# Attention inside a split-precision matmul kernel: the products of weights and values, three steps back to back in place of two

## The chip, the cores and the metric

One core of a Trainium2 chip. The time is that of the device for one launch, in microseconds (us); a time of a kernel is the median of its runs. A profiled execution is one such run whose instructions were recorded. Engines are called PE (matrix), ACT (scalar), DVE (vector), POOL (GpSimd) and SP (which only issues DMAs here).

## The reference

Three layers follow each other. All is float32.

```python
# attention: q, k, v are (4 batches, 8 heads, 576 positions, 64)
scores = q @ k.T / 8 + bias          # bias: -slope * distance
mask = (rel >= 0) & (rel < 128)      # a query sees itself and the 127 keys before it
attn = softmax(where(mask, scores, -1e9))
x = attn @ v                         # -> (2304 tokens, 512)
# first block: 512 -> 1536 -> 512
x = (sigmoid(x @ w_gate) * (x @ w_val)) @ w_out
# second block: 512 -> 1024 -> 1024 -> 512
y = ((x @ w1) * (x @ w2)) @ w3 @ moe2_w_out
```

The kernel multiplies `w3` by `moe2_w_out` first (the fold), so that the second block ends in one product.

## The kernel before

**The dense work.** Tokens are taken in three thirds of 768. Every factor is split into a high and a low part in a reduced float format, and a product is three matmuls in that format (lines 610 to 612: high by high, low by high, high by low). Each weight matrix comes in groups of 256 columns, 6 groups for the first block and 4 for the second, so 30 groups in all. A group is multiplied by seven products in place of eight (P1 to P7, issued in the order P1, P5, P6, P2, P7, P3, P4; each is 6 matmuls), whose results DVE puts together in four pieces C11, C22, C12, C21. PE's work after the head is a list of 90 **sections**, numbered 0 to 89 here: `gate` and `val` for each group (the seven products with the gate weights, then with the value weights), and `proj` (or `pair0` and `pair1` at a block's end), in which the hidden result of the group before is multiplied by the output weights, in tiles of 6 matmuls. Within a block the sections run gate, val, gate, val, proj, gate, val, proj, and so on: sections 2, 5, 8, 11, 14 are gates, 3, 6, 9, 12, 15 vals, 4, 7, 10, 13 projs.

**The attention.** It is cut into 80 steps of 128 queries (some of 64) of two heads. A step n passes through a chain over all engines: `scores(n)` on PE (line 633), `score` on DVE, `exponentials` on ACT, `reciprocals` on DVE, `normalise` on POOL, `turn(n)` on PE, which turns the weights (line 648), `turned_copy(n)` into the place `pt[n % 2]` (DVE in the head, ACT later), `pv(n)` on PE (line 668), the product of turned weights and values, and `out_copies` on ACT (line 810) into the token matrix `xf`. The first 28 steps (`HEAD`) run in a head of 32 **slots** beside the fold, a step in each slot: scores(s), turn(s - 3). The other 52 run inside sections: step 28 + sec has its scores at the start of section sec, is turned in section sec + 1 (after P5, or after the second tile).

**Where pv stands.** Two steps are multiplied at a time. In the head pv(n - 1) and pv(n) stand at the start of slot n + 4 for odd n, and in the sections pv(m - 1) and pv(m) in section m + 1 - 28 for odd m, after P7 or after the sixth tile. So every even section holds a pair. The matmuls of pv are plain float32 and use 64 columns of the array for each of the two heads; all others use 128. A step of 64 queries also uses 64 rows of the array in half of its matmuls. The trace shows each float32 matmul of pv and scores as two instructions, so a full pair is 16.

**What it waits for.** In the sections `attn[0]` is the bank for scores and for the results of pv, so scores(n) waits for the copies of the pair before (`x_ready`), and ACT makes them in its own order: in a gate section between the pieces C11 and C22 of the gate, in a val section after the first `hidden_hi`. In a gate section ACT's chain is exponentials, turned_copy, `out_hi` (the output weights' high part, which waits for a DMA), a table load for the sigmoid, then gate(C11). P1 of the val section behind it waits for gate(C11), since they share a bank.

**DVE in a val section** makes the results and the hidden pieces in a fixed order, result_21 (line 1055) last, which is followed by hidden(C21), and its low part; the third tile of a proj or pair0 section waits for what stands at the end of that order.

**SP** issues all loads in program order. `load_v(j)` waits until the pv that read the old values is done, and whatever is behind it waits too.

## Time and profile before

| | |
|---|---|
| median of 3 runs | 885.34 us (883.81 to 888.36) |
| the profiled execution | 886.31 us |
| its span, first to last instruction | 884.5 us |
| PE busy | 864.6 us, 98% of the span |
| DVE, ACT, POOL busy | 515.2, 475.0, 594.9 us |
| matmuls of pv (line 668) | 576 instructions, in 40 groups |

The profiled execution took 0.97 us more than the median. The span lacks 1.8 us of it, which lie around the program. PE is granted full clock from about 22 us on. Its matmuls overlap, so a small wait doesn't show as idle time; what a piece of PE's work takes is read from the starts of the instructions around it.

### The profile page before, as it was taken

How to read it: one execution, taken by the hardware profiler on the slowest of the kernel's cores; microseconds unless marked ns; L12 is line 12 of the kernel's file. 1: busy time of each engine (PE TensorE's matmuls, PEld its weight loads, DVE VectorE, ACT ScalarE, POOL GpSimd, SP SyncE). 2: the span in 40 equal slices, each digit the busy share in tenths (PEclk: the TensorE clock that was granted, in tenths of full speed). 3: DMA queues.
4: the chain of work that ended last, by engine and by line, in shares of the span. 5: the costliest groups of instructions: out<-in, count | busy, mean ns of one | idle time of the engine just before them, and what ended most of it. 6: DMA issues, size and time to landing. Idle time of an engine off the chain costs nothing.

```text
span 884.5 us, 15389 instructions
## 1 busy us (share of the span) xinstructions
PE 864.6 (98%) x5272; PEld 825.7 (93%) x5272; DVE 515.2 (58%) x1209; ACT 475.0 (54%) x1043; POOL 594.9 (67%) x502
## 2 busy tenths in 40 slices
PE   5999999999999999999999999999999999999998
PEld 4887899999999999999999999999999999999998
DVE  5464656555467646656456656555676555576554
ACT  5566575666655644668555575633544444445330
POOL 3449588666655986758766663896859866738930
PEclk8999999999999999999999999999999999999999
DMA  8465323304222133331332122222221222212202
GB/s 243 123 197 161 113 93 103 92 15 117 91 79 82 35 104 98 100 126 52 96 109 88 48 81 80 72 72 72 80 102 46 84 72 72 72 49 72 72 24 73
DMA packets 59453, 78.79 MB, mean 89 GB/s; under 512 B 23152, under 2 KB 40688, under 8 KB 59376
## 3 DMA queue, kind: packets, MB, share of 16 engines
q1 hardware_dynamic: 58432, 77.52, 27.8%
q8 instruction: 43, 0.70, 0.3%
q10 hardware_dynamic: 944, 0.30, 0.1%
q14 instruction: 34, 0.28, 0.1%
HBM read 70.98 MB, written 6.82 MB: 88 GB/s over the span
## 4 chain that ended last, share of the span: by engine, by line
PE 80%; DVE 4%; ACT 4%; POOL 4%; issue 3%; DMA 2%; SPq 1%; ACTq 0%; DVEq 0%; POOLq 0%
PE quad_ps L610 14%; PE quad_ps L612 13%; PE quad_ps L611 13%; PE o_ps L610 11%; PE o_ps L612 10%; PE o_ps L611 10%; PE attn_ps L668 4%; PE attn_ps L633 3%; PE attn_ps L648 2%; DMA wo_lo_raw<-w_out 1%; DVE h_lo L1071 1%; PE quad_ps L633 1%; PE quad_ps L648 1%; POOL wq_lo L1280 1%; POOL wq_lo L1273 1%
## 5 line engine op out<-in xcount | busy, mean ns | idle before, releaser
L610 PE MATMUL quad_ps<-xs_hi,wq_hi 128*128 128x384 f32 x840 | 291.6, 347 | 3.2 <-DVE quad_ps L1043 1.8
L612 PE MATMUL quad_ps<-xs_hi,wq_lo 128*128 128x384 f32 x840 | 281.5, 335 | 0.0
L611 PE MATMUL quad_ps<-xs_lo,wq_hi 128*128 128x384 f32 x840 | 281.3, 335 | 0.0
L610 PE MATMUL o_ps<-h_hi,wo_hi 128*128 128x384 f32 x480 | 166.3, 347 | 3.0 <-DVE h_lo L1071 2.4
L610 PEld LDWEIGHTS quad_ps<-xs_hi,wq_hi 128*128 128x128 f32 x840 | 157.8, 188 | 10.3 <-issue 3.9
L612 PE MATMUL o_ps<-h_hi,wo_lo 128*128 128x384 f32 x480 | 161.3, 336 | 0.0
L611 PE MATMUL o_ps<-h_lo,wo_hi 128*128 128x384 f32 x480 | 161.1, 336 | 0.0
L611 PEld LDWEIGHTS quad_ps<-xs_lo,wq_hi 128*128 128x128 f32 x840 | 158.0, 188 | 0.0
L612 PEld LDWEIGHTS quad_ps<-xs_hi,wq_lo 128*128 128x128 f32 x840 | 157.7, 188 | 0.0
L1236 POOL TENSOR_TENSOR soft<-soft,recip 128x384 f32<-128x384 f32 (+2 forms) x80 | 58.3, 729 | 145.4 <-DVE recip L985 145.3
L1280 POOL TENSOR_TENSOR wq_lo<-wsum,wq_hi 128x1024 fp32r<-128x1024 f32 x60 | 144.3, 2405 | 8.5
L1273 POOL TENSOR_TENSOR wq_lo<-raw_q,wq_hi 128x768 fp32r<-128x768 f32 x60 | 110.7, 1845 | 52.4 <-ACT wq_hi L834 52.4
L1082 DVE TENSOR_TENSOR xf<-o_ps,xf 128x384 f32<-128x384 f32 x144 | 80.0, 556 | 65.9 <-PE o_ps L612 64.3
L1032 DVE TENSOR_TENSOR u<-quad_ps,s 128x384 f32<-128x384 f32 x60 | 33.4, 557 | 138.6 <-PE quad_ps L612 138.6
L868 ACT CAST h_hi<-quad_ps 128x384 fp32r<-128x384 f32 x120 | 57.6, 480 | 101.6 <-DVE quad_ps L1066 101.6
L610 PEld LDWEIGHTS o_ps<-h_hi,wo_hi 128*128 128x128 f32 x480 | 90.1, 188 | 8.5 <-issue 8.3
L611 PEld LDWEIGHTS o_ps<-h_lo,wo_hi 128*128 128x128 f32 x480 | 90.2, 188 | 0.0
L612 PEld LDWEIGHTS o_ps<-h_hi,wo_lo 128*128 128x128 f32 x480 | 90.1, 188 | 0.0
L848 ACT COPY s<-quad_ps 128x384 f32<-128x384 f32 x60 | 28.8, 481 | 110.5 <-PE quad_ps L612 110.5
L1286 POOL TENSOR_TENSOR wo_lo<-wo_lo_raw,wo_hi 128x1024 fp32r<-128x1024 f32 x30 | 71.6, 2394 | 19.2 <-ACT wo_hi L842 19.2
L797 ACT ACTIVATE soft<-soft,negmax 128x192 f32<-128x192 f32 (+1 forms) x144 | 62.0, 432 | 36.0 <-DVE negmax L975 35.8
L860 ACT ACTIVATE sig<-quad_ps 128x384 f32<-128x384 f32 x120 | 57.0, 495 | 35.0 <-DVE quad_ps L1049 14.7
(68 smaller groups left out, 1365.4 us busy)
## 6 DMA issues: line engine op xcount, KB each, us to landing
raw_q<-w SPq DMA_DIRECT2D x24, 512.0 KB, 3.7
raw_q<-w_gate SPq DMA_DIRECT2D x18, 512.0 KB, 3.6
raw_q<-w_val SPq DMA_DIRECT2D x18, 512.0 KB, 4.6
wo_lo_raw<-w_out SPq DMA_DIRECT2D x18, 512.0 KB, 4.2
wo_lo_raw<-w_times_wout SPq DMA_DIRECT2D x12, 512.0 KB, 3.8
w_raw<-w3t SPq DMA_DIRECT2D x16, 256.0 KB, 3.2
outT<-xf SPq DMA_DIRECT2D x8, 384.0 KB, 3.8
q_sb<-qT SPq DMA_DIRECT2D x30, 96.0 KB, 3.5
```

The costliest lines, as they stand in the source:

```text
L610: pe.matmul(out, lh, rh, start=start, stop=False, skip_group_check=onto)
L611: pe.matmul(out, lh, rl, start=False, stop=False, skip_group_check=onto)
L612: return pe.matmul(out, ll, rh, start=False, stop=stop, skip_group_check=onto)
L633: mm = pe.matmul(score_cols(n, u), q_sb[st][:, w], k_sb[st][:, keys], start=True, stop=True)
L797: op = nc.scalar.activation(soft_cols(n, u), soft_cols(n, u), ACT.Exp, scale=-1.0, bias=negmax[:, at + u:at + u + 1], accum_out=rowsum[:, ...
L860: nc.scalar.activation(sig[:, piece(blk)], quad[BANK_OUT[blk]][:, 0:TH], func).then_inc(gated, 1)
L868: nc.scalar.copy(h_hi[g % 2][:, piece(blk)], quad[BANK_OUT[blk]][:, 0:TH]).then_inc(h_hi_done, 1)
L1082: op = nc.vector.tensor_tensor(out=place, in0=ps_o[t % 2][:, 0:TH], in1=place, op=ALU.add)
L1236: nc.gpsimd.tensor_tensor(out=cols, in0=cols, in1=recip[:, at:at + units].unsqueeze(2).to_broadcast([P, units, UW - lo]), op=ALU.mult).the ...
L1273: nc.gpsimd.tensor_tensor(out=wq_lo[m][:, 0:PLAIN], in0=raw_q[m][:, GW:GW + PLAIN], in1=wq_hi[m][:, 0:PLAIN], op=ALU.subtract).then_inc(wq ...
L1280: nc.gpsimd.tensor_tensor(out=wq_lo[m][:, PLAIN:7 * GW], in0=wsum[m][:, :], in1=wq_hi[m][:, PLAIN:7 * GW], op=ALU.subtract).then_inc(wq_sp ...
L1286: nc.gpsimd.tensor_tensor(out=wo_lo[g % 2][:, :], in0=wo_raw[g % 2][:, :], in1=wo_hi[g % 2][:, :], op=ALU.subtract).then_inc(wo_split, 1)
```

## The change

pv is issued for three steps at a time. The new lists `VALUES` (the groups of three, counted anew from step 28, the last group of each stretch with one step) say which, and where: a group stands in the slot or section in which its last step's pv stood before. A third buffer `pt` holds turned weights. In the head a group has a bank of its own, alternating; in the sections its three results lie side by side in `attn[0]`. ACT's `out_copies` copies three, and SP's `load_v` stands where its group of three is done.

```diff
+VALUES = [list(range(a, min(a + 3, end))) for lo, end in ((0, HEAD), (HEAD, NSTEP)) for a in range(lo, end, 3)]
+VALUES_AT = {ns[-1]: i for i, ns in enumerate(VALUES)}
+VALUES_OF = {n: i for i, ns in enumerate(VALUES) for n in ns}
...
-        pt = [sb(ctx, f"pt{b}", [P, 4 * P], F32) for b in range(2)]
+        pt = [sb(ctx, f"pt{b}", [P, 4 * P], F32) for b in range(3)]
...
-            bank, start = (attn[n % 2], 0) if n < HEAD else (attn[0], n % 2 * 2 * UW)
+            bank = attn[VALUES_OF[n] % 2] if n < HEAD else attn[0]
+            start = (n - VALUES[VALUES_OF[n]][0]) * P
...
-                    if s == end_of(before(j, v_set)) + LAG_PV:
+                    if s == values_end(before(j, v_set)) + LAG_PV:
                         load_v(j)
...
-                    if end_of(before(j, v_set)) > HEAD and sec == end_of(before(j, v_set)) + 1 - HEAD:
+                    if end_of(before(j, v_set)) > HEAD and sec == values_end(before(j, v_set)) + 2 - HEAD:
                         load_v(j)
...
-                    pe.wait_ge(x_ready, n - 1 if n == HEAD else (n - 1) // 2 * 2)
+                    pe.wait_ge(x_ready, VALUES[VALUES_OF[n - 1]][0])
...
-                if 0 <= s - LAG_PV < HEAD and s % 2:
-                    pv(s - LAG_PV - 1)
-                    pv(s - LAG_PV)
+                if s - LAG_PV in VALUES_AT:
+                    for n in VALUES[VALUES_AT[s - LAG_PV]]:
+                        pv(n)
...
-                        if j == P7 and m is not None and m % 2:
-                            pv(m - 1)
-                            pv(m)
+                        if j == P7 and m in VALUES_AT:
+                            for n in VALUES[VALUES_AT[m]]:
+                                pv(n)
...
-                for n in (last - 1, last):
+                for n in VALUES[VALUES_AT[last]]:
                     nc.scalar.copy(out_cols(n), pv_cols(n)).then_inc(x_ready, 1)
...
-                wait(act, pv_done, n - 1)
-                nc.scalar.copy(cols(pt[n % 2]), cols(turn_bank(n))).then_inc(pt_done, 1)
+                wait(act, pv_done, n - 2)
+                nc.scalar.copy(cols(pt[n % 3]), cols(turn_bank(n))).then_inc(pt_done, 1)
```

The waits of pv itself follow: in the head for the copies two groups back, in the sections for those of the group before and for DVE's reading of the scores that share the bank.

On PE in the head, slots 5 and 6: before, the first two steps are multiplied (`attn_ps<-pt,v_sb`) in slot 5, after the scores (`quad_ps<-k_sb,q_sb`) and ahead of the transposes (`quad_ps<-eye,soft`).

```order
L633 MATMUL quad_ps<-k_sb,q_sb 128x192
L668 MATMUL attn_ps<-pt,v_sb 64x128 x6
L648 MATMUL quad_ps<-eye,soft 128x128 x4
L610 MATMUL o_ps<-wo_hi,w_hi 128x512
L611 MATMUL o_ps<-wo_lo,w_hi 128x512
```

Now slot 5 goes from scores to transposes:

```order
L645 MATMUL quad_ps<-k_sb,q_sb 128x192
L660 MATMUL quad_ps<-eye,soft 128x128 x4
L622 MATMUL o_ps<-wo_hi,w_hi 128x512
L623 MATMUL o_ps<-wo_lo,w_hi 128x512
L624 MATMUL o_ps<-wo_hi,w_lo 128x512
L645 MATMUL quad_ps<-k,q 128x64
L645 MATMUL quad_ps<-k,q 128x128
L681 MATMUL attn_ps<-pt,v_sb 64x128 x10
L660 MATMUL quad_ps<-eye,soft 128x128 x4
```

and three steps stand in slot 6. From there a group comes every third slot.

On ACT in sections 2 to 4 (gate, val, proj of the second group): `sig` is the gate's pieces, `h_hi` the hidden ones, `pt` the turned copy, `xf<-attn_ps` the copies of pv's results. Before:

```order
L860 ACT_TABLE_LOAD
L860 ACTIVATE sig<-quad_ps 128x384
L810 COPY xf<-attn_ps 128x128 x2
L860 ACTIVATE sig<-quad_ps 128x384 x3
L848 COPY s<-quad_ps 128x384
...
L836 CAST wq_hi<-wsum 128x1024
L868 CAST h_hi<-quad_ps 128x384 x3
...
L836 CAST wq_hi<-wsum 128x1024
L810 COPY xf<-attn_ps 128x128 x2
```

and now:

```order
L873 ACT_TABLE_LOAD
L873 ACTIVATE sig<-quad_ps 128x384 x4
L861 COPY s<-quad_ps 128x384
...
L849 CAST wq_hi<-wsum 128x1024
L881 CAST h_hi<-quad_ps 128x384
L823 COPY xf<-attn_ps 128x128 x3
L881 CAST h_hi<-quad_ps 128x384 x2
```

The copies left the gate section and the proj section and stand in the val section between them, as pv does on PE. This goes on: groups stand in sections 3, 6, 9, up to 51, and one of a single step in 52, where pairs stood in 2, 4, 6, up to 52. In the first block all of them are val sections.

## Rows read from the trace of the kernel before

**Rows 1.** PE in order: start us, length us, engine, line, operation, count; section 8.

```profile
177.83 0.34 PE L612 MATMUL quad_ps<-xs_hi,wq_lo 128*128 128x384 f32 x1
...
179.41 0.33 PE L611 MATMUL quad_ps<-xs_lo,wq_hi 128*128 128x384 f32 x1
```

**Rows 2.** PE in order, around a pair of 12 instructions, section 16.

```profile
253.06 0.34 PE L612 MATMUL o_ps<-h_hi,wo_lo 128*128 128x384 f32 x1
...
254.42 0.34 PE L611 MATMUL o_ps<-h_lo,wo_hi 128*128 128x384 f32 x1
```

**Rows 3.** PE in order: pairs with a step of 64 queries, sections 26 and 32.

```profile
345.19 1.03 PE L668 MATMUL attn_ps<-pt,v_sb 128*64 128x128 f32 x16
...
402.34 1.18 PE L668 MATMUL attn_ps<-pt,v_sb 128*64 128x64 f32 x16
```

**Rows 4.** PE in order, head: a slot without a pair, one with it.

```profile
44.78 0.49 PE L633 MATMUL quad_ps<-k,q 128*128 128x192 f32 x2
...
45.24 0.48 PE L610 MATMUL o_ps<-wo_hi,w_hi 128*128 128x512 f32 x1
...
61.75 0.49 PE L633 MATMUL quad_ps<-k,q 128*128 128x192 f32 x2
...
63.38 0.48 PE L610 MATMUL o_ps<-wo_hi,w_hi 128*128 128x512 f32 x1
```

**Rows 5.** PE in order, third tile of sections 4, 13 and 46; in brackets idle time and releaser.

```profile
136.78 0.41 PE L610 MATMUL o_ps<-h_hi,wo_hi 128*128 128x384 f32 x1
...
221.18 0.60 PE L648 MATMUL attn_ps<-eye,soft 128*128 128x128 f32 x4
221.53 0.42 PE L610 MATMUL o_ps<-h_hi,wo_hi 128*128 128x384 f32 x1
...
526.63 0.60 PE L648 MATMUL attn_ps<-eye,soft 128*128 128x128 f32 x4
527.61 0.41 PE L610 MATMUL o_ps<-h_hi,wo_hi 128*128 128x384 f32 x1 [0.39 <-DVE h_lo L1071]
```

**Rows 6.** DVE in order: result_21 at the end of sections 12 and 45.

```profile
219.13 0.55 DVE L1055 TENSOR_TENSOR quad_ps<-quad_ps,u 128x384 f32<-128x384 f32 x1
...
525.86 0.56 DVE L1055 TENSOR_TENSOR quad_ps<-quad_ps,u 128x384 f32<-128x384 f32 x1
```

**Rows 7.** PE in order: scores and the first product or tile behind, sections 7, 12.

```profile
162.20 0.81 PE L633 MATMUL attn_ps<-k_sb,q_sb 128*128 128x192 f32 x4
162.71 0.47 PE L610 MATMUL o_ps<-h_hi,wo_hi 128*128 128x384 f32 x1
...
208.48 0.81 PE L633 MATMUL attn_ps<-k_sb,q_sb 128*128 128x192 f32 x4
...
209.35 0.41 PE L610 MATMUL quad_ps<-xs_hi,wq_hi 128*128 128x384 f32 x1
```

**Rows 8.** SP and ACT in order: loads of section 10 and 11, ACT in section 11.

```profile
197.78 0.38 SPq L480 DMA_DIRECT2D v_sb<-v  x1
...
200.29 0.33 SPq L513 DMA_DIRECT2D wo_lo_raw<-w_out  x1
...
206.35 1.05 ACT L842 CAST wo_hi<-wo_lo_raw 128x1024 fp32r<-128x1024 f32 x1 [2.20 <-DMA wo_lo_raw<-w_out]
```

**Rows 9.** ACT and PE in order: the end of section 2.

```profile
124.33 0.49 ACT L860 ACTIVATE sig<-quad_ps 128x384 f32<-128x384 f32 x1
...
125.30 0.68 PE L633 MATMUL attn_ps<-k_sb,q_sb 128*128 128x64 f32 x4 [0.22 <-ACT xf L810]
125.73 0.42 PE L610 MATMUL quad_ps<-xs_hi,wq_hi 128*128 128x384 f32 x1
```

**Rows 10.** ACT and PE in order: sections 8 and 9.

```profile
178.01 0.49 ACT L860 ACTIVATE sig<-quad_ps 128x384 f32<-128x384 f32 x1
...
181.69 0.42 PE L610 MATMUL quad_ps<-xs_hi,wq_hi 128*128 128x384 f32 x1
```

**Rows 11.** PE in order, head, slot 28: a fold that waits.

```profile
81.13 0.50 PE L610 MATMUL o_ps<-wo_hi,w_hi 128*128 128x512 f32 x1 [0.59 <-POOL w_lo L1297]
```

More of the change, by code:

```diff
@@ L218, in starts_batch, with values_end @@
     return JOBS[j][3] == 0 and i == 0
+VALUES = [list(range(a, min(a + 3, end))) for lo, end in ((0, HEAD), (HEAD, NSTEP)) for a in range(lo, end, 3)]
+VALUES_AT = {ns[-1]: i for i, ns in enumerate(VALUES)}
+VALUES_OF = {n: i for i, ns in enumerate(VALUES) for n in ns}
+def values_end(j):
+    return VALUES[VALUES_OF[end_of(j) - 1]][-1]
 def chunks_of(n):
@@ L656, in pv @@
                 pe.wait_ge(pt_done, n + 1)
+                steps = VALUES[VALUES_OF[n]]
                 if n < HEAD:
-                    wait(pe, x_ready, n - 1)
+                    wait(pe, x_ready, VALUES[VALUES_OF[n] - 1][0] if VALUES_OF[n] else 0)
                 else:
-                    pe.wait_ge(x_ready, n // 2 * 2)
-                    pe.wait_ge(scored, min(n // 2 * 2 + 3, NSTEP))
+                    pe.wait_ge(x_ready, steps[0])
+                    pe.wait_ge(scored, min(steps[-1] + 2, NSTEP))
                 for c in chunks_of(n):
                     rows = slice(0, rows_of(n) if c == 1 else P)
-                    right = pt[n % 2][rows, c * 2 * P:(c + 1) * 2 * P].rearrange("p (u h n) -> p u h n", u=2, h=2)
+                    right = pt[n % 3][rows, c * 2 * P:(c + 1) * 2 * P].rearrange("p (u h n) -> p u h n", u=2, h=2)
                     for h in range(2):
@@ L785, in _ @@
                             turn(m)
-                        if i == 5 and m is not None and m % 2:
-                            pv(m - 1)
-                            pv(m)
+                        if i == 5 and m in VALUES_AT:
+                            for n in VALUES[VALUES_AT[m]]:
+                                pv(n)
         @block.scalar
@@ L882, in _ @@
             for s in range(SLOTS + 1):
-                if 0 <= s - LAG_PV - 1 < HEAD and s % 2 == 0:
+                if s - LAG_PV - 1 < HEAD and s - LAG_PV - 1 in VALUES_AT:
                     out_copies(s - LAG_PV - 1)
@@ L931, in _ @@
                     gate(g, C11)
-                    if m is not None and m % 2:
+                    if m in VALUES_AT:
                         out_copies(m)
@@ L939, in _ @@
                     hidden_hi(g, C11)
-                    if m is not None and m % 2:
+                    if m in VALUES_AT:
                         out_copies(m)
@@ L948, in _ @@
                         weights_hi(g + 1, 1)
-                    if m is not None and m % 2:
+                    if m in VALUES_AT:
                         out_copies(m)
@@ L955, in _ @@
                     x_hi(inst, P5)
-                    if m is not None and m % 2:
+                    if m in VALUES_AT:
                         out_copies(m)
@@ L960, in _ @@
                 else:
-                    if m is not None and m % 2:
+                    if m in VALUES_AT:
                         out_copies(m)
@@ L990, in turned_copy @@
                 dve.wait_ge(turned, n + 1)
-                wait(dve, pv_done, n - 1)
-                nc.vector.tensor_copy(cols(pt[n % 2]), cols(turn_bank(n))).then_inc(pt_done, 1)
+                wait(dve, pv_done, n - 2)
+                nc.vector.tensor_copy(cols(pt[n % 3]), cols(turn_bank(n))).then_inc(pt_done, 1)
             def fold_copy(m):
```

## The prediction, made before the changed kernel had run

> **What bounds the kernel now.** First the busy shares: PE is busy in 98% of the span, every other engine in 67% or less (the table above), so the time is PE's own work and the few places at which it waits. Then PE in order of time, and in it the distance from one start to the next, because matmuls overlap and the idle time in brackets shows only a part of a wait. The dense products start every 0.17 us without a break; the reader is to look for the larger distances. They are of two kinds. One kind stands at both ends of each group of pv, always of the same size. The other comes where PE waits for DVE, ACT or POOL, in different sizes, and depends on where a pair of pv gives the other engines time. The change touches both: there are 28 groups in place of 40, and most of them stand elsewhere.
>
> **A group's fixed price in the sections.** From the last product before a pair of 16 instructions to the second product behind it are 1.58 us [rows 1]; two ordinary distances of 0.17 would be 0.35, so the pair costs 1.23. A pair of 12 takes 1.36 [rows 2], so 1.01. The difference, 0.22 for four instructions, is 0.055 for each; 16 of them are 0.88, and 0.35 remain that don't depend on how many there are. Of these 0.10 lie ahead of the group and the rest inside its start, at its end, and at the product behind. Groups in sections fall from 26 to 18: 8 x 0.35 = 2.8 us less. All of it is PE's own time and nothing hides it. The Trainium skill speaks against this term: its page "TensorE: Matmul & The Clock Gate", section "Step-by-step: what each phase is for", says that the engine pulls weight loads ahead of the matmuls in flight, so that one matmul should follow another without a gap. By that page of the Trainium skill alone a group would have no price of its own, and without this term and its part in the head the sum would be 882.9. The Trainium skill's page "TensorEngine Tiling (Array Packing)", section "Key Properties", says on the other side that changing the tiling mode drains the engine, and pv is the only work in 64 columns.
>
> **In the head.** From scores to the first fold are 0.46 us without a pair (44.78 to 45.24) and 1.63 with one of 16 (61.75 to 63.38) [rows 4]; less 0.88 that leaves 0.29, say 0.3 for each group. They fall from 14 to 10.
>
> **Steps of 64 queries** cost more where another step follows in the group: 1.18 against 1.03 us [rows 3], 0.15. Of the 16 such steps 8 were last in their pair, and 6 are last in their group of three (or alone): two more pay, one in the head and one in the third third, 0.3 us.
>
> **Waits behind val sections.** In the third tile of a proj or pair0 section PE waits for the end of DVE's order. Where the val section held a pair, four transposes and the next product start 0.35 apart (221.18 to 221.53); in section 46, behind a val section without one, 0.98 (526.63 to 527.61), so the wait is 0.63. There are seven such, in sections 4, 10, 16, 28, 34, 40 and 46, from 0.32 in the first (136.78) to 0.63 in the last, together 2.6 us [rows 5]. The cause is a backlog of DVE: result_21 starts 2.05 us ahead of the transposes in the one (219.13) and 0.77 ahead in the other (525.86) [rows 6]. pv gives PE something to do after P7, while DVE catches up. Now each of the seven val sections in front holds a group of three, which gives more time than a pair. The backlog that would have to be left for a wait to return is 1.3 us; I take all 2.6 us as gone. What ACT adds in such a section is one more copy (two fit between the gate piece's end at 124.82 and the scores that wait for them at 125.30 [rows 9], so at most 0.24 us for one), behind the group and ahead of two hidden pieces, and P3 and P4 (12 x 0.17 = 2.1 us) hide it.
>
> **Waits at the start of val sections.** P1 waits for the gate piece C11 in sections 6, 12 and 36. In section 12 scores and product start 0.87 apart in place of 0.51 [rows 7]: 0.36. The other two, read in the same way, are 0.09 and 0.58; together 1.0 us. ACT was late because the output weights came late: it waited 2.20 us for them [rows 8]. SP had issued the new values at 197.78, when pv of its own section was done (in the others it waits for the section before), and the loads behind them, gate weights and output weights, went out together, so that the latter took 6.1 us from 200.29 to 206.35. Now every load of values waits for a group in the section before SP's place, in this place and in the two like it. I take the 1.0 us as gone.
>
> **What is lost: the cover in gate sections.** Nine gate sections held a pair and hold none now: 2, 8, 14, 20, 26, 32, 38, 44 and 50. There the pair's 1.23 us lay between ACT's gate C11 and the P1 that waits for it. In section 8 the piece ends at 178.50 and P1 starts at 181.69, 3.2 us later [rows 10]: without the pair 2.0 remain. In 14, 20, 26, 38, 44 and 50 the same reserve, from 1.7 to 4.1 us, also covers 1.23, in section 50 barely. Not in the sections after a block's start, 2 and 32, where ACT is behind: the piece ends at 124.82, P1 starts at 125.73 [rows 9], a reserve of 0.9. In section 2 PE also waits 0.39 now for the copies ahead of scores (125.30 [rows 9], read from the starts as above), and this wait goes. So PE would come 1.23 + 0.39 = 1.6 us earlier, and 0.7 of it is waited for again, 0.9 with 0.15 for the handing over: a loss of 0.5 against now. In section 32 the same sum gives 1.3 - 0.9 + 0.15 = 0.5. Together 1.0 us.
>
> **The head as a whole.** Up to slot 28 four groups are saved (12 to 8), 1.2 us, less 0.15 for a step of 64 queries. But there a fold waits for POOL [rows 11], which has worked almost without a break since slot 22 and won't be earlier because PE is; it starts its run on scores that come about 1.2 us earlier (three groups of 0.3, less 0.15, and one step's pv, 8 x 0.055, that now stands later). So the head gains 1.1 or 1.2 us, not more; 1.1 is taken. It could be nothing if POOL's run starts with a load or with ACT.
>
> **Two edits with one answer.** The third `pt` place and the other bank columns add no instruction. The loads of values are as many as before and come up to two steps later, with at least two groups between a load and the product that needs it; PE waits for none now.
>
> **The sum.** -2.8 (sections) + 0.15 (one step of 64 queries; the other is in the head's term) - 2.6 - 1.0 + 1.0 - 1.1 = -6.4 us. The profiled execution, 886.31, would be 879.9; it lies 0.97 above the median of 885.34, so the forecast is **878.9 us**, 0.7% less.
>
> **The rivals.** (a) Only the fixed price goes. The waits behind val sections move on to something else that is late at the same place (ACT, which has three copies, or POOL's low parts), and only 2.8 + 1.1 - 0.15, less the 1.0 lost, come: -2.8, 882.6 us. For it speaks that the waits are small against chains of several engines; against it that sections 7, 13, 25, 37 and 43, which already follow a val section with a pair, show none. (b) The gate sections lose their cover altogether. If the output weights still come late, as in section 11, the sigmoid ends just before P1 in each of the nine sections, and all of the pair's 1.23 us is waited for: 11 us in place of the 1.0 above, so 878.9 + 10 = 889 us, slower. It decides from the point at which the weights land 2 us later than they do in section 8. Against it speaks that the loads there are issued in the same order after the change as before. (c) More goes than I count: in section 52 the transposes wait 0.6 us for POOL, and a longer section 51 may cover it; in the head PE also waits for a copy of the pair before, and now waits for older ones. All of it together is -8.0, 877.3 us.
>
> **How the numbers follow.** The forecast with its neighbours (c) has 0.72, (a) 0.22, (b) 0.06. The range holds (a) and (c) with one us for the runs' own spread (the three of before lie between -1.5 and +3.0 of their median): 876 to 883.2. About 0.5%, 4.4 us, is what a measurement of this kernel can tell from no change. The forecast lies 6.4 below, (a) 2.8: faster 0.72, within 0.5% 0.23, slower 0.05.
>
> **What would show it.** 28 groups of pv, each with 0.35 us of its own: a group of 24 instructions should take 0.35 + 24 x 0.055 = 1.67 us between products. The third tiles of sections 4, 10, 16, 28, 34, 40 and 46 start 0.14 or 0.35 behind the transposes. P1 of sections 6, 12 and 36 starts 0.51 after scores; P1 of sections 3 and 33 waits 0.5 to 0.9, which no section did there before. The fold in slot 28 still waits for POOL. I am wrong if waits of that kind stand in the sections 9, 15, 21, 27, 39, 45 or 51 too (the cover was worth more than I read), or if the third tiles still wait for DVE (the backlog isn't what pv clears), or if a group of three costs more at its ends than a pair.

## The result, and the profile after

The changed kernel takes 879.61 us (median of 6 runs, 877.91 to 879.99), against 885.16 for the kernel before (6 runs). The medians lie 5.6 us apart. The ratio is 0.9934, with a 95% interval of 0.992 to 0.9948, so 0.7% less and clear of no change. The profiled execution took 879.99 us, its span is 878.2. A second set of runs of the same kernel gave 0.9927 (0.9911 to 0.9944).

The page of the profile shows the same picture as the one before: one engine that works, four that wait for it. Columns: busy us, share of the span, instructions.

```profile
span 878.2 us, 15386 instructions
...
PE 859.5 (98%) x5272; PEld 826.8 (94%) x5272; DVE 518.0 (59%) x1209; ACT 475.9 (54%) x1043; POOL 595.7 (68%) x502
```

PE's busy time fell by 5.1 us while its instructions are the same in number. Part of that is overlap at the edges of the groups, and part is waits that were too short to show as idle time. So the account is made from starts, as in the prediction. I read three stretches in each trace: the head up to the first product of section 0, sections 0 to 52, and the rest.

| stretch | before | after | forecast |
|---|---|---|---|
| head | 98.00 | 97.14 | -1.1 |
| sections 0 to 52 | 492.24 | 486.68 | -5.3 |
| sections 53 to 89 and the end | 294.27 | 294.37 | 0 |

**A group of 24** in section 3 (PE in order of time: start us, length us, engine, line, operation, count). Line 681 is pv, and 622 to 624 are the products.

```profile
129.68 0.34 PE L624 MATMUL quad_ps<-xs_hi,wq_lo 128*128 128x384 f32 x1
129.94 1.53 PE L681 MATMUL attn_ps<-pt,v_sb 128*64 128x128 f32 x24
131.41 0.44 PE L622 MATMUL quad_ps<-xs_hi,wq_hi 128*128 128x384 f32 x1
131.69 0.34 PE L623 MATMUL quad_ps<-xs_lo,wq_hi 128*128 128x384 f32 x1
```

From the last product ahead of the group (129.68) to the second one behind it (131.69) are 2.01 us. Less 0.35 that is 1.66; the prediction had 1.67. The first three rows are those of [rows 1] with eight instructions more. The price at the edges is that of a pair.

**Third tiles** of sections 4, 13 and 46, which answer to [rows 5]:

```profile
136.35 0.38 PE L660 MATMUL attn_ps<-eye,soft 128*128 128x128 f32 x2
136.49 0.42 PE L622 MATMUL o_ps<-h_hi,wo_hi 128*128 128x384 f32 x1
...
219.18 0.60 PE L660 MATMUL attn_ps<-eye,soft 128*128 128x128 f32 x4
219.54 0.42 PE L622 MATMUL o_ps<-h_hi,wo_hi 128*128 128x384 f32 x1
...
522.13 0.60 PE L660 MATMUL attn_ps<-eye,soft 128*128 128x128 f32 x4
522.48 0.42 PE L622 MATMUL o_ps<-h_hi,wo_hi 128*128 128x384 f32 x1
```

Four transposes and the tile start 0.35 or 0.36 apart, two transposes and the tile 0.14. None of the seven waits is left. On DVE, result_21 ahead of section 4 starts at 134.29, 2.06 us ahead of the transposes at 136.35:

```profile
134.29 0.55 DVE L1068 TENSOR_TENSOR quad_ps<-quad_ps,u 128x384 f32<-128x384 f32 x1
```

This is the distance of [rows 6] behind a val section with a pair, 2.05 us. DVE has caught up in the same way.

**P1 of sections 3, 9 and 12.** The prediction named the first as a new wait, the second as one that is covered, the third as one that goes. The ACT row is gate piece C11 of section 8.

```profile
122.78 0.61 PE L645 MATMUL attn_ps<-k_sb,q_sb 128*128 128x64 f32 x4
124.10 0.41 PE L622 MATMUL quad_ps<-xs_hi,wq_hi 128*128 128x384 f32 x1 [0.71 <-ACT sig L873]
...
176.94 0.49 ACT L873 ACTIVATE sig<-quad_ps 128x384 f32<-128x384 f32 x1
...
179.00 0.61 PE L645 MATMUL attn_ps<-k_sb,q_sb 128*128 128x64 f32 x4
179.36 0.42 PE L622 MATMUL quad_ps<-xs_hi,wq_hi 128*128 128x384 f32 x1
...
206.55 0.81 PE L645 MATMUL attn_ps<-k_sb,q_sb 128*128 128x192 f32 x4
207.07 0.47 PE L622 MATMUL quad_ps<-xs_hi,wq_hi 128*128 128x384 f32 x1
```

Scores of 64 queries and P1 are 0.36 apart where nothing is waited for (section 9) and 1.32 in section 3, so PE waits 0.96 there for the gate piece C11. In section 12 the distance is 0.52, against 0.87 in [rows 7].

**The head** still ends behind POOL, with 0.89 us of wait in slot 28 against 0.83 in [rows 11]:

```profile
80.11 0.50 PE L622 MATMUL o_ps<-wo_hi,w_hi 128*128 128x512 f32 x1 [0.64 <-POOL w_lo L1310]
```

### The profile page after: what moved, and what is told of

Its sections match the earlier page's. It is cut to its first block, busy times and chain, and to the rows that moved or that the text cites. A ratio compares the mean times of both kernels' runs of the same rounds, so it can differ in the third digit from the quotient of the medians.

```text
span 878.2 us, 15386 instructions
## 1 busy us (share of the span) xinstructions
PE 859.5 (98%) x5272; PEld 826.8 (94%) x5272; DVE 518.0 (59%) x1209; ACT 475.9 (54%) x1043; POOL 595.7 (68%) x502
## 4 chain that ended last, share of the span: by engine, by line
PE 87%; DVE 3%; POOL 3%; ACT 2%; issue 2%; DMA 1%; SPq 1%; DVEq 0%; ACTq 0%; POOLq 0%
PE quad_ps L622 15%; PE quad_ps L624 14%; PE quad_ps L623 14%; PE o_ps L622 11%; PE o_ps L624 11%; PE o_ps L623 11%; PE attn_ps L681 4%; PE attn_ps L645 3%; PE attn_ps L660 2%; PE quad_ps L645 1%; PE quad_ps L660 1%; DVE h_lo L1084 1%; POOL wq_lo L1293 1%; DMA wo_lo_raw<-w_out 1%; DMA w_raw<-w3t 1%
```

## The experiments

All variants start from one of the two kernels, or from another variant, and change one thing; only the two versions at the end change several on purpose. Beside the median and its ratio to the kernel before, which ran on the same chip, the table has the stretch from P1 of section 3 to P1 of section 53. It leaves out the head and the first three sections, and repeats well where the code is the same: 464.5 and 464.5 in the two kernels whose sections are those of before (the kernel before, and the variant that changes only the head), 459.7, 459.9 and 459.7 in the three that share the changed sections (the changed kernel twice, and head_four). A median resolves about 1 us here, the stretch 0.2.

| kernel | groups in sections | median us | ratio (95%) | sections 3 to 52, us |
|---|---|---|---|---|
| before | 26 | 885.16 | 1 | 464.5 |
| changed | 18 | 879.61 | 0.9934 (0.9920 to 0.9948) | 459.7 |
| split | 35 | 883.55 | 0.9981 (0.9971 to 0.9992) | 465.0 |
| groups in gate | 18 | 883.75 | 0.9983 (0.9973 to 0.9994) | 463.6 |
| groups in proj | 18 | 883.36 | 0.9979 (0.9968 to 0.9991) | 463.6 |
| head only | 26 | 884.14 | 0.9989 (0.9978 to 1.0001) | 464.5 |
| load later | 26 | 884.55 | 0.9993 (0.9981 to 1.0005) | 463.8 |
| full columns | 18 | 905.13 | 1.0222 (1.0202 to 1.0243) | 476.5 |
| sections four | 13 | 880.78 | 0.9950 (0.9932 to 0.9967) | 461.8 |
| head four | 18 | 879.21 | 0.9936 (0.9917 to 0.9956) | 459.7 |
| gate, DVE swapped | 18 | 883.69 | 0.9981 (0.9969 to 0.9994) | 464.0 |
| mixed | 18 | 879.60 | 0.9932 (0.9916 to 0.9947) | 459.8 |
| changed again | 18 | 879.40 | 0.9927 (0.9911 to 0.9944) | 459.9 |
| out first | 18 | 879.18 | 0.9923 (0.9907 to 0.9939) | 458.7 |

### Has a group a price of its own?

```diff
                         if j == P7 and m in VALUES_AT:
-                            for n in VALUES[VALUES_AT[m]]:
+                            for n in VALUES[VALUES_AT[m]][:2]:
+                                pv(n)
+                        if j == P3 and m in VALUES_AT:
+                            for n in VALUES[VALUES_AT[m]][2:]:
                                 pv(n)
```

> The changed kernel, but in the 17 sections that hold a group of three the first two steps stand after P7 (or the sixth tile) as now and the third stands one product later, after P3 (in proj sections such groups don't occur; the gate sections 18, 30 and 48 are split in the same way). Same section, same instructions, same copies: only the number of groups rises, from 18 to 35 in the sections. If a group has a price of its own of 0.35 us, as read from the kernel before: 17 x 0.35 = 6.0 us more than the changed kernel, 885.6 us, with 0.2 us less if steps of 64 queries become last. If a group has no price of its own, and what I read is the price of something else around it, the time stays at 879.6. The third tiles behind should still not wait, since pv still stands in the val section.

PE in order of time, section 3 of this variant:

```profile
127.95 0.34 PE L624 MATMUL quad_ps<-xs_hi,wq_lo 128*128 128x384 f32 x1
128.22 1.09 PE L681 MATMUL attn_ps<-pt,v_sb 128*64 128x128 f32 x16
...
129.53 0.33 PE L623 MATMUL quad_ps<-xs_lo,wq_hi 128*128 128x384 f32 x1
...
130.23 0.34 PE L624 MATMUL quad_ps<-xs_hi,wq_lo 128*128 128x384 f32 x1
130.50 0.66 PE L681 MATMUL attn_ps<-pt,v_sb 128*64 128x128 f32 x8
...
131.37 0.34 PE L623 MATMUL quad_ps<-xs_lo,wq_hi 128*128 128x384 f32 x1
```

The two parts take 129.53 - 127.95 - 0.35 = 1.23 and 131.37 - 130.23 - 0.35 = 0.79 us, together 2.02 where the group in one took 1.66. So the second group costs 0.36 us and does no work for it. Summed over all groups of the sections pv takes 33.0 us against 27.7, which is 5.3 for 17 groups. The stretch grew by 5.2. The 0.7 less than my 6.0 are steps of 64 queries: in four sections (18, 27, 39 and 48), where one becomes the last of its part, the split costs 0.20 in place of 0.36. I had put 0.2 for all of them. The median rose by 0.47% of the kernel before, 4.2 us, less than the trace's 5.3 but within the two intervals. The third tiles behind don't wait, as expected. A group has a price, and it is 0.35 us.

### Is it the number of groups, or their place?

In the changed kernel the first group of the sections is made shorter, and so all later ones move by one section. The number of groups stays.

```diff
-VALUES = [list(range(a, min(a + 3, end))) for lo, end in ((0, HEAD), (HEAD, NSTEP)) for a in range(lo, end, 3)]
+VALUES = [list(range(a, min(a + 3, HEAD))) for a in range(0, HEAD, 3)] + [[HEAD, HEAD + 1]] + [
+    list(range(a, min(a + 3, NSTEP))) for a in range(HEAD + 2, NSTEP, 3)]
```

> The changed kernel with the first group of the sections holding two steps in place of three, so that every later group stands one section earlier: in gate sections 2, 5, 8, ... 50 (17, 29 and 47 are pair1 sections), never in a val section of them. Still 18 groups in the sections, same instructions. If the cover in val sections is what removed the waits of third tiles: in the kernel before nine val sections without a pair had waits of 0.29 us behind them on average; 17 of them give 4.9 us; the waits of P1 in sections 3 and 33 (1.5 us in the changed kernel) go, since gate sections have their cover again: 879.6 + 4.9 - 1.5 = 883.0 us. If only the number of groups counts, 879.6. If the cover in gate sections was worth more than I read, the time is below 879.6.

With `[[HEAD]]` and `HEAD + 1` in the new lines the groups stand in the proj sections.

> The changed kernel with the first group of the sections holding one step, so that every later group stands in the section behind: proj sections 4, 7, 10, ... (pair0 for 16, 28, 46; val for 1, 19, 31, 49). Still 18 groups in the sections. Neither val nor gate sections have a cover: third tiles wait after nearly all val sections (14 x 0.29 = 4.1 us or more), P1 of sections 3 and 33 waits as in the changed kernel: 879.6 + 4.1 = 883.7 us, and it should be slower than the variant with groups in gate sections by some 0.7 us or more. If only the number of groups counts, 879.6.

By the medians they gave back 4.1 and 3.8 us of the changed kernel's gain. The expectations were 883.0 and 883.7; that the second would be 0.7 us slower isn't seen, for the stretch is 463.6 in both. What waits is what was named. PE in the variant with groups in gate sections, third tile of section 46:

```profile
521.70 0.60 PE L661 MATMUL attn_ps<-eye,soft 128*128 128x128 f32 x4
522.69 0.41 PE L623 MATMUL o_ps<-h_hi,wo_hi 128*128 128x384 f32 x1 [0.39 <-DVE h_lo L1085]
```

It is the wait of [rows 5] again, to 0.01 us: 0.99 from transposes to tile. Ten third tiles wait in this variant (sections 4, 7, 10, 13, 16, 28, 34, 37, 43 and 46; not 22, 25, 40 and 52), 3.2 us together; I had expected 17 waits with 4.9. P1 of sections 3 and 33 no longer waits. There are two waits that I had not expected. At the start of the second and third block (sections 18 and 48) a product waits 0.9 us for DVE, because the group that gave DVE time there now stands a section earlier:

```profile
269.84 0.34 PE L625 MATMUL quad_ps<-xs_hi,wq_lo 128*128 128x384 f32 x1
270.89 0.41 PE L623 MATMUL quad_ps<-xs_hi,wq_hi 128*128 128x384 f32 x1 [0.71 <-DVE quad_ps L1057]
```

So the sum came out nearly right (883.0 against 883.7) with two of its terms wrong: the waits behind val sections were 1.7 us too many, those at the block starts were missing. In the variant with groups in proj sections the last turn, in section 52, waits 1.7 us for POOL, and the turns of sections 22 and 34 wait 1.0 and 0.6 for it, which I had not expected either. P1 of sections 3 and 33 waits 0.7 and 0.3 there, less than the 0.96 and 0.52 of the changed kernel. So here, too, the sum came out right with terms that were wrong.

### The head alone

```diff
+VALUES = [list(range(a, min(a + 3, HEAD))) for a in range(0, HEAD, 3)] + [[a, a + 1] for a in range(HEAD, NSTEP, 2)]
```

> Groups of three in the head alone; in the sections pairs and load_v stand as in the kernel before. The traces put the head's share at 0.9 us, so 884.3 us. If part of the sections' gain was made in the head (POOL or the loads starting earlier and so the waits of the sections changing), it would be below 883.

884.14 us, and the stretch is that of the kernel before (464.54 against 464.51). The sections' gain isn't made in the head. The head itself varies between profiles of one code: from the scores of step 4 to P1 of section 0 it took 77.8 and 77.3 us in the two profiles with pairs (the kernel before and the variant "load later"), and 75.7 to 76.7 in those with threes, full columns left out.

Most of this is the granted clock. It was 0.50 of full, the lower of its two levels (1.2 GHz), from 16.5 to 23.3 us in the profile of the kernel before, where PE had just waited 1.8 us for POOL, and from 16.2 to 23.0 in that of the changed one. Of this 3.1 and 2.6 us lie behind the scores of step 4. In "load later" and in the changed kernel's second profile this part is 1.9 us, and in eight other profiles it is nothing. The rest is a wait for POOL in slot 23, 0.15 to 0.20 us in most profiles with threes and 0.44 to 0.71 in three (split, groups in proj, gate with DVE swapped). So profiles have to be compared at the same clock: with 1.9 us of half clock in both, pairs take 77.26 and threes 76.41, which puts the head's gain at 0.85 us. The first comparison had 0.9, and the median of this variant is 0.8 lower than that of the kernel before beside it. The same shows in whole runs. In the four sets of runs of the kernel before that stand beside the variants, those with a mean granted clock of 1.0 have a median of 884.4 us (39 runs), those with 0.998 one of 886.1 (28 runs).

### The load of values

The kernel before, with one edit: a load that had to wait for the pair of its own section is issued one section later.

```diff
-                    if end_of(before(j, v_set)) > HEAD and sec == end_of(before(j, v_set)) + 1 - HEAD:
+                    if end_of(before(j, v_set)) > HEAD and sec == end_of(before(j, v_set)) // 2 * 2 + (
+                            end_of(before(j, v_set)) % 2) * 2 + 1 - HEAD:
```

> The kernel before, with one edit: the three loads of values that waited on SP for a pair of their own section (sections 4, 10, 34) are issued one section later, as in the changed kernel. Everything else stands as before. If these loads are what made the output weights late: P1 of sections 6, 12 and 36 starts 0.51 us behind scores in place of 0.60, 0.87 and 1.09, the sections' time falls by 1.0 us and the median to about 884.1. If the waits of P1 there come from ACT's other work, they stay and so does the time.

ACT in section 11 and PE at the start of section 12:

```profile
203.10 0.56 ACT L817 COPY pt<-attn_ps 128x512 f32<-128x512 f32 x1
203.57 1.05 ACT L842 CAST wo_hi<-wo_lo_raw 128x1024 fp32r<-128x1024 f32 x1
...
208.00 0.81 PE L633 MATMUL attn_ps<-k_sb,q_sb 128*128 128x192 f32 x4
208.51 0.47 PE L610 MATMUL quad_ps<-xs_hi,wq_hi 128*128 128x384 f32 x1
```

The cast of the output weights follows at once, where it had waited 2.20 us in [rows 8], and P1 starts 0.51 behind scores. Sections 6 and 36 show the same 0.51. The cause is shown. The stretch fell by 0.7 us, not 1.0: some sections are 0.04 to 0.07 longer, which I didn't follow up. The median can't tell this from nothing.

### Where the 0.35 us come from

```diff
-                        left = key_chunk(n, c) * P + h * D
-                        mm = pe.matmul(pv_cols(n)[h * D:(h + 1) * D, :].rearrange("p (u n) -> p u n", n=U),
-                                       v_sb[st][rows, left:left + D], right[:, 0:units, h, :],
-                                       start=c == chunks_of(n)[0], stop=c == 1)
+                        left = key_chunk(n, c) * P
+                        mm = pe.matmul(pv_cols(n)[:, :].rearrange("p (u n) -> p u n", n=U),
+                                       v_sb[st][rows, left:left + P], right[:, 0:units, h, :],
+                                       start=h == 0 and c == chunks_of(n)[0], stop=h == 1 and c == 1)
```

> The changed kernel, but each matmul of pv takes the values of both heads, 128 columns, and writes 128 rows of the bank; which head a row belongs to is not kept apart, so x is another one. Same number of instructions, same places, same type (plain float32), same waits. If the price of a group (0.35 us) is that of changing from 128 columns to 64 and back, it falls to 0.1 or less: 28 groups x 0.25 = 7 us less, 872.6 us. If it comes from the change of type, or from the group's own first loads and results, the edges stay as they are and the time is 879.6 give or take 1.

PE in sections 3 and 6, a group of 24 and one of 20:

```profile
138.53 0.33 PE L624 MATMUL quad_ps<-xs_hi,wq_lo 128*128 128x384 f32 x1
138.70 2.84 PE L681 MATMUL attn_ps<-pt,v_sb 128*128 128x128 f32 x24
...
141.55 0.34 PE L623 MATMUL quad_ps<-xs_lo,wq_hi 128*128 128x384 f32 x1
...
167.29 0.33 PE L624 MATMUL quad_ps<-xs_hi,wq_lo 128*128 128x384 f32 x1
167.46 2.39 PE L681 MATMUL attn_ps<-pt,v_sb 128*128 128x128 f32 x20
...
169.86 0.34 PE L623 MATMUL quad_ps<-xs_lo,wq_hi 128*128 128x384 f32 x1
```

24 instructions take 141.55 - 138.53 - 0.35 = 2.67 us, 20 take 2.22. The difference is 0.11 for each, and 24 x 0.11 is the whole 2.67: nothing is left for the edges. PE starts the group 0.17 behind the product, as any other, and no longer 0.26. So the price was that of going to 64 columns and back. What it consists of can be read in the changed kernel, from the weight loads of PE (PEld) around the group of section 3:

```profile
129.50 0.19 PEld L624 LDWEIGHTS quad_ps<-xs_hi,wq_lo 128*128 128x128 f32 x1
129.94 1.29 PEld L681 LDWEIGHTS attn_ps<-pt,v_sb 128*64 128x64 f32 x24 [0.25 <-issue]
131.40 0.19 PEld L622 LDWEIGHTS quad_ps<-xs_hi,wq_hi 128*128 128x128 f32 x1 [0.17 <-issue]
```

The weights of the last product are loaded from 129.50 on and its matmul starts at 129.68, 0.17 later: the load runs during the matmul ahead. At both edges of the group it doesn't. The first load of pv starts at 129.94 with its matmul, and the first load behind at 131.40 with the matmul of 131.41. In full columns the first load of the group again starts 0.17 ahead of its matmul.

But the time rose to 905.13, 25.5 us above the changed kernel, where I had expected 7 less, for the traces also show what the 64 columns give: an instruction costs 0.11 us in full columns and 0.055 in half of them. The two heads stand next to each other in the order and use different halves of the array, and their matmuls overlap: within a group of the changed kernel the starts come in pairs 0.007 us apart, a pair every 0.109 us, while in full columns there is one start every 0.112. 576 instructions x 0.057 are 32.7 us more, 28 groups x 0.35 are 9.8 less, together +22.9; 25.5 were measured. At least part of the rest is in the steps of 64 queries, which still change the rows of the array: in section 27, with one such step, the 20 instructions take 2.51 us in place of 2.22. I had written down only the second term.

The Trainium skill ("TensorEngine Tiling (Array Packing)", "Key Properties") says both things, that a change of the tiling mode drains the engine and that different tiles work in parallel. The trace agrees, with 0.35 us for a change there and back and 0.055 against 0.11 us for an instruction. The pulling ahead of weight loads, which the prediction cited against this term, is seen only where the mode stays the same: 0.17 us of lead there, none at the two edges.

### Four steps to a group

In the sections: four places for turned weights, and `range(a, min(a + 4, NSTEP))` from `HEAD` on in steps of four.

> The changed kernel with four steps to a group in the sections (13 groups in place of 18, at sections 4, 8, 12, ... 48, 52, whatever their kind) and four places for turned weights; the head keeps its threes. If time is the sum of a price for each group and of the waits that the cover decides: 5 x 0.35 = 1.75 us less, and the waits of third tiles behind val sections without a group come back as in the variant with groups in gate sections (4, 7, 10, 16, 28, 34, 43, 46: 2.6 us), P1 in section 33 no longer waits (0.5): 879.6 - 1.75 + 2.6 - 0.5 = 880.0 us, no gain. If only the number of groups counts, 877.9.

880.78 us, and the stretch is 2.1 us longer than with threes, although pv is 1.8 us cheaper (25.9 against 27.7). That fewer groups alone would count is out. Waits at the third tile or the transposes ahead of it are back in the eight sections named (4, 7, 10, 16, 28, 34, 43 and 46), 2.8 us in all where I had 2.6; P1 of section 33 doesn't wait, 0.5 less. What I had missed is the last turn:

```profile
574.10 0.34 PE L625 MATMUL o_ps<-h_hi,wo_lo 128*128 128x384 f32 x1
576.06 0.44 PE L661 MATMUL attn_ps<-eye,soft 128*128 128x128 f32 x2 [1.63 <-POOL soft L1250]
```

It waits 1.8 us for POOL's normalised weights, 1.7 more than in the changed kernel, whose section 51 holds a group and so is 1.7 us longer. -1.8 + 2.8 - 0.5 + 1.7 = 2.2, and 2.1 were found.

In the head: four steps to a group there, with four places for turned weights and the two banks of the results swapped, and threes in the sections.

```diff
+VALUES = [list(range(a, min(a + 4, HEAD))) for a in range(0, HEAD, 4)] + [
+    list(range(a, min(a + 3, NSTEP))) for a in range(HEAD, NSTEP, 3)]
```

> The changed kernel with four steps to a group in the head (7 groups in place of 10, at slots 7, 11, 15, 19, 23, 27, 31), four places for turned weights, and ACT's first two copies of x one slot later. The sections keep their threes. PE has 3 x 0.3 = 0.9 us less to do in the head. If the fold in slot 28 is bound by POOL, whose run doesn't start earlier, the head ends 0.3 us earlier at most and the wait there grows from 0.9 to 1.2 or more: 879.3 us. If the head is PE's time alone, 878.7, and the wait at slot 28 stays at 0.9.

879.21 us, 0.9936: no difference from threes that can be told. PE late in the head (line 661 is the turn):

```profile
67.92 0.81 PE L646 MATMUL quad_ps<-k_sb,q_sb 128*128 128x192 f32 x4
68.97 0.66 PE L661 MATMUL quad_ps<-eye,soft 128*128 128x128 f32 x4 [0.24 <-POOL soft L1250]
...
72.18 0.66 PE L661 MATMUL quad_ps<-eye,soft 128*128 128x128 f32 x4 [0.70 <-POOL soft L1250]
...
78.78 0.50 PE L623 MATMUL o_ps<-wo_hi,w_hi 128*128 128x512 f32 x1 [0.52 <-POOL w_lo L1311]
```

PE waits for POOL earlier, in two turns (0.4 and 0.9 us), and at the fold a little less (0.76) than before, not more as I had written. POOL is the bound here. Its first sum of weights (`wsum`) starts 46.1 us behind the scores of step 4, no earlier than in the profiles with threes at full clock (45.7 to 46.3), and PE meets POOL where it arrives first. From the scores of step 4 to P1 of section 0 are 76.4 us, all at full clock. The threes at full clock take 75.7 to 76.3, so four steps to a group gain nothing.

### What DVE's lateness is

In the variant with groups in gate sections, in proj sections:

```diff
                 elif kind == "proj":
+                    add_up(e, 0)
                     if n is not None:
                         score(n)
-                    add_up(e, 0)
                     hidden(g, C21)
```

> The variant with the groups in gate sections, and on DVE in every proj section the first tile is added up ahead of the attention's score in place of behind it; nothing else is moved. In that variant the third tiles of sections 4, 7, 10, 13, 34, 37 and 43 start 0.25 to 0.33 us late, because they need the bank that DVE empties with the first tile. If they are late because DVE is behind, by 0.55 us of score just ahead, these seven waits go, 2.0 us: 881.7 us against 883.7. Sections 16, 28 and 46 (pair0) keep theirs. If the waits come from the hidden pieces and not from the first tile, nothing changes.

883.69 us, no change, and the stretch is 0.4 us longer. The third tiles of the seven sections no longer wait (section 37 keeps 0.05 us), and yet nothing is gained. PE in section 4:

```profile
132.96 0.38 PE L661 MATMUL attn_ps<-eye,soft 128*128 128x128 f32 x2
133.10 0.42 PE L623 MATMUL o_ps<-h_hi,wo_hi 128*128 128x384 f32 x1
...
134.07 0.34 PE L625 MATMUL o_ps<-h_hi,wo_lo 128*128 128x384 f32 x1
134.32 0.41 PE L623 MATMUL o_ps<-h_hi,wo_hi 128*128 128x384 f32 x1
```

The tile starts 0.14 behind two transposes, where it started 0.45 behind them. The fourth tile is late in its place: it starts 0.25 behind the product ahead of it, where 0.17 is usual. The seven sections are between 0.14 us shorter and 0.19 longer than in the variant without the edit, and section 22, which had no wait, is 0.21 longer. DVE has the same work in the same time, and what is put ahead of one piece makes another late. This one change of order doesn't remove the backlog, which speaks for a backlog of DVE as a whole; other orders weren't tried. Time on PE does remove it, and pv, which has to be done anyway, gives that time.

### Two versions made from the readings

The first puts groups of two back into gate sections 2 and 32 and groups of four into 6 and 36, and has the edit on DVE.

```diff
+FROM = [*range(0, HEAD, 3), 28, 30, *range(34, 58, 3), 58, 60, *range(64, NSTEP, 3)]
+VALUES = [list(range(a, b)) for a, b in zip(FROM, FROM[1:] + [NSTEP])]
```

> A version made from the readings. The changed kernel with four places for turned weights, groups of two in gate sections 2 and 32 (where the loss of the cover cost 0.96 and 0.52 us), of four in val sections 6 and 36, none in 3 and 33, all others as they are, so still 18 groups; and DVE adds up the first tile ahead of the score in proj sections, so that the third tiles of sections 4 and 34 don't wait for it. The two waits of P1 go (1.5 us) and scores of section 3 wait again for two copies (0.4): 1.1 us less than the changed kernel, 878.5 us. If the order of DVE doesn't carry the third tiles, 0.6 us of that is lost again.

> The changed kernel itself once more, for comparison with the two others on the same chip: 0.9934 of the kernel before, 879.6 us.

879.60 against 879.40 us on the same chip. The two waits of P1 are gone, but sections 4, 7, 10, 13, 22, 34 and 43, all with the edit on DVE, are 0.2 us longer each, and the stretch is the same, 459.8. Its profile also shows a wait of 2.0 us for P1 of section 1, where the changed kernel has 0.5 and 0.7 in its two profiles:

```profile
101.38 1.05 ACT L856 CAST wo_hi<-wo_lo_raw 128x1024 fp32r<-128x1024 f32 x1 [2.10 <-DMA wo_lo_raw<-w_out]
...
104.37 0.41 PE L623 MATMUL quad_ps<-xs_hi,wq_hi 128*128 128x384 f32 x1 [1.68 <-ACT sig L874]
```

It is the chain of [rows 8] again. SP issued two loads of the second group's weights at 91.45 and 91.93 and the output weights behind them at 94.12; they landed at 101.38, 7.3 us later. This wait is between 0.2 and 2.0 us in the profiles of the variants so far, so it can be part of what runs differ by.

The second version leaves DVE as it was and issues the output weights first.

```diff
+            load_out(0)
             load_quad(1, 0)
```

> The mixed version without its edit on DVE, and with one on SP: the first output weights are loaded ahead of the two quads of the second group's weights, not behind them. P1 of section 1 waits for a chain that starts with this load (5.7 us to land in the changed kernel, 7.3 us in the mixed version, beside the two other loads); alone it should land in 3.7, as such loads do on average, so the wait of 0.5 to 2.0 us there goes, and P1 of section 2 doesn't wait in its place, since POOL takes the quads up 9 us after they were issued. Third tiles of sections 4 and 34 wait 0.3 each again, third tiles of 7, 13 and 22 don't lose what they lost to the edit on DVE (0.2 each in 6 sections). Against the changed kernel: P1 of sections 3 and 33 1.5 less, scores of section 3 0.4 more, third tiles 0.6 more, P1 of section 1 0.7 less: 878.4 us. If the loads behind now come too late, section 2 waits and the time is 879.5 or more.

SP, ACT and PE up to P1 of section 1:

```profile
96.04 0.33 SPq L526 DMA_DIRECT2D wo_lo_raw<-w_out  x1
...
101.09 1.03 ACT L858 CAST wo_hi<-wo_lo_raw 128x1024 fp32r<-128x1024 f32 x1
...
103.80 0.81 PE L648 MATMUL attn_ps<-k_sb,q_sb 128*128 128x192 f32 x4
104.32 0.47 PE L625 MATMUL quad_ps<-xs_hi,wq_hi 128*128 128x384 f32 x1
```

The output weights landed 3.5 us after their issue, the two loads behind them 4.4 and 5.5 after theirs. They no longer make ACT wait, and P1 starts 0.52 behind scores; P1 of section 2 doesn't wait. P1 of sections 3 and 33 doesn't wait, and the third tiles of sections 4 and 34 do, 0.3 each. The stretch is 458.7, 1.1 us less than the changed kernel's, and the best of all. The median is 879.18 and the ratio 0.9923 (0.9907 to 0.9939), against 0.9934 and 0.9927 for the changed kernel in two sets. The mechanisms are shown by the trace; that this version is faster than the changed kernel isn't shown by the times, whose intervals overlap.

## Why the prediction was right

878.9 was forecast, 879.6 measured. The span fell by 6.3 us where the sum had 6.4. That alone would say little, for sums agree by luck; so term by term, from the two traces:

| term | forecast | read after |
|---|---|---|
| fixed price in the sections, with one step of 64 queries | -2.65 | -2.5 |
| waits behind val sections | -2.6 | -2.6, all seven gone |
| P1 of sections 6, 12 and 36 | -1.0 | -1.0, all gone |
| cover lost in gate sections | +1.0 | +1.1 (section 3: 0.96 - 0.39, section 33: 0.52), and 0.1 in section 51 |
| head | -1.1 | -0.9 in this pair of profiles |
| not in the sum: last turn, section 52 | | -0.5 |
| not in the sum: a product of section 29 | | -0.35 |

In the sections the terms that were read come to -5.8, and -5.6 was found. That the total was met to 0.1 us is partly luck: the terms of the sum gave about 0.6 us less than forecast, head included, and 0.85 us came from two places that were not in it.

**The fixed price** held in size, and the two experiments on it give its cause: 0.36 us for a group more in the split, none for a group in full columns. The prediction left open what happens at the two ends. The weight loads show it: they lose their lead there.

**The waits behind val sections** went for the reason given. The places decide, since 18 groups in other places gave back about 4 of the 5.6 us. Of the seven waits, that of section 40 had been only 0.04 us. But the reason was put too narrowly. I took a val section without pv to be followed by a wait of a certain size, and carried this over to val sections which had always held a pair: 17 waits of 0.29, where 10 came, 3.2 us in all. And I read the end of DVE's order as the thing that PE waits for, while in the proj sections it is the bank that DVE empties with the first tile. When that piece was moved ahead another was late. Both errors cost nothing in the forecast, whose seven waits were read one by one, and both cost me in the experiments.

**The loads** were right in cause and in place, shown by the variant that moves them alone.

**The lost cover** was right to 0.1 us for each of the two sections: 0.57 and 0.52 against 0.5 and 0.5. The other seven gate sections kept their reserve. In section 9 P1 starts 1.93 us behind the end of the gate piece, where the prediction had left 2.0. Section 50 was called barely covered, and PE waits 0.13 there. The rival of 889 us, in which the output weights come late in every gate section, didn't happen because each load of values now waits for a pv long done.

**Rival (c)**, more gain than counted, was partly true: the last turn waits 0.12 us in place of 0.63. That is what made up for the head, which gave 0.2 less than forecast. **Rival (a)**, in which the waits move on to something else, is out.

**The head** is the weakest term. Its mechanism is confirmed, since four steps to a group gave nothing more and PE waits for POOL all the same. Its size was set too high: at the same granted clock pairs and threes differ by 0.85 us, where the term had 1.1. Without that comparison the size would be lost in the profiles, since the head of one code differs by 1 us between them.

## What to carry to other kernels

Work of another tiling mode has a price at each group of it, read as the difference between a long group and a short one; put it together, but ask first what the old places were giving to the others. Here the number of groups brought 2.5 us in the sections, and their places with the later loads of values another 3.1; the same 18 groups in other places gave 3.9 of it back, and a longer group in the wrong place gave back more than it saved. A wait behind an engine that has fallen behind went when the engine that waits was given other work; the one change of order that was tried on the late engine only moved the wait to the next piece. Before the starts of two profiles are compared, their granted clocks should be. And where an experiment takes away a price, write down also what the price was paying for.

## What the runs showed of the hardware

- Changing from 128 to 64 columns and back costs PE 0.35 us, 0.10 of it ahead of the first matmul. With pv in 128 columns both edges vanish in groups whose steps all have 128 queries (changed kernel and full columns, sections 3 and 6).
- A weight load starts 0.17 us ahead of its matmul in a row of products, and not ahead of it at either change (changed kernel, section 3).
- Two float32 matmuls in different halves of the columns overlap: 0.055 us for an instruction, against 0.11 in full columns.
- A load of 512 KB of output weights lands in 3.7 us as a rule (the page of the changed kernel). Behind two others of the same size it took 5.7 us (changed kernel, section 0) and 7.3 us (mixed version); issued ahead of both it took 3.5 (out first).
- The clock granted to PE near the start differs between executions of one kernel. It was 0.50 of full from 16.2 to 23.0 us in one profile of the changed kernel and from 18.3 to 21.7 in the other, and full from there on.
